# Attention and two MLPs on one core: the first product of each MLP as seven block products per pair of tiles

## The chip, the core and the metric

The kernel runs on one core of one Trainium2 chip. The core has TensorE (PE in the rows, its weight loads apart as PEld), VectorE (DVE), ScalarE (ACT), GpSimd (POOL) and SyncE (SP, which here only starts DMAs). They share the on-chip memory SBUF; TensorE writes its results to PSUM, eight banks of 512 fp32 columns, which DVE and ACT read. The metric is the device time of one launch in microseconds; lower is better.

## What is computed

Attention over 4 x 8 heads of 576 tokens with rotary positions gives x, 2304 tokens by 512. Two MLPs follow, each with 2048 hidden features:

```python
def _moe_ref(x, w_in, w_out, s, b):
    h = x @ w_in                 # 2304x512 @ 512x2048
    r = np.maximum(h, 0.0)
    g = s * (r * r) + b
    return (g @ w_out).astype(np.float32)

def _moe2_ref(x, w_in, w_out):
    h = x @ w_in
    g = h * (1.0 / (1.0 + np.exp(-1.702 * h)))
    return (g @ w_out).astype(np.float32)
```

All is fp32. Every product of the MLPs is made of three TensorE products: an operand is split in a high part (rounded to the type fp32r, which TensorE reads) and a low part (the rest), and high x high, high x low and low x high are summed in PSUM.

## The kernel before

Every engine has its own program, written out by hand, and engines wait for each other on counting semaphores. The attention of 16 pairs of heads comes first. Tables (PE_ORDER, ACT_ORDER, DVE_ORDER, POOL_ORDER, SP_ORDER) set the order of its steps on each engine; "H@-1" means that step H of pair p stands in round p + 1. A hook `after(s)` of the SP and POOL programs puts further work behind round s; that is where the first weights are loaded (L275, L277) and split (`first_w`, L309 and L288).

The MLPs then run in 192 steps, n = 0 to 191. The 2304 tokens are cut in six chunks C of 384, and for every chunk of every MLP there are 16 steps, one for each 128 hidden features. The attention's result and later the first MLP's lie transposed in `xT`, as four tiles of 128 features. A step has on TensorE:

- `H_step` (L956): 4 input tiles x 3 products = 12 matmuls of 384 columns into one of two PSUM banks (`hps`).
- `Y_step` (L984), two steps later (LAG = 2): in the first MLP 4 x 3 = 12 matmuls of 384 columns, in the second 3 x 3 = 9 of 512 columns, summed over the chunk's 16 steps in banks ACC. Chunks take turns on these banks.

Between the two, `gate` on ACT and `gate_low` on DVE apply the function and split the result in `ghi` and `glo`: relu or sigmoid (L918, L920), square or product (L932, L934), high part (L924, L926), low part (L937, L940). `extras` adds what comes seldom: weights are split once for each MLP (`split_w`, L285 on ACT, L288 on DVE) and kept in SBUF for all six chunks; the next chunk's x is split in steps 5, 7, 9 and 11 (`split_x`, L294 and L297), one tile of 384 each, into the other of two buffers; `evacuate` (L997, L1000) copies a chunk's result to `xT`. GpSimd has nothing to do in the MLPs: it splits the first two weights and the low part of the first x during the attention and ends with `finish` (L538, L542, L545), which normalises a pair's result and writes it to `xT`. Step 0 of H stands inside the last round of the attention, between the two PV products (L651) of the last pair.

## Time and profile before

| | us |
|---|---|
| median of 3 runs | 1119.11 |
| lowest, highest | 1119.0, 1119.51 |
| span of the profiled execution | 1117.4 |

Busy time in the profiled execution: TensorE matmuls 1090.4 us (98%), weight loads 1036.1 (93%), DVE 553.5 (50%), ACT 500.8 (45%), POOL 247.4 (22%). The profiled execution's span runs from the first to the last instruction; the device time is 1.7 us longer. Matmuls overlap in the pipeline, so a row's duration of a matmul says little; what counts is the distance between the starts of two of them. The attention takes the first 315 us, the MLPs the rest, and the trace gives for each instruction its start, its length and, where its engine was idle before, what released it.

### The profile page before, as it was taken

To read this page: it belongs to the slowest core of one execution; us is meant where nothing else is said; L and a number is where in the kernel's file an instruction comes from. 1 tells how busy PE (TensorE), PEld (TensorE's weight loads), DVE (VectorE), ACT (ScalarE), POOL (GpSimd) and SP (SyncE) were. 2 spreads that over 40 slices of the span, in tenths; PEclk is the share of its full clock that TensorE was granted. 3 is DMA by queue.
4 is the path that set the end of the run, shared out by engine and by line. 5 is a ranking of instruction groups with operands and counts; after the bars stand their busy time and mean duration, and the time that the engine had idled before them with its cause. 6 is when DMAs were issued, how large, how long until landed. Compare 5 with 4: busy or idle time off the path is not lost.

```text
span 1117.4 us, 16936 instructions
## 1 busy us (share of the span) xinstructions
PE 1090.4 (98%) x6522; PEld 1036.1 (93%) x6522; DVE 553.5 (50%) x885; ACT 500.8 (45%) x1031; POOL 247.4 (22%) x276
## 2 busy tenths in 40 slices
PE   4899999999999999999999999999999999999998
PEld 4899999999999999999999999999999999999997
DVE  6888888898866333333333356532332323333222
ACT  4888788878755332232332345422322222222222
POOL 6878878895720000000000000000000000000000
PEclk9999999999999999999999999999999999999999
DMA  4555454553243100000000014200000000000000
GB/s 109 126 147 145 128 152 130 147 138 91 69 132 125 37 1 1 1 1 1 1 1 1 1 57 133 76 1 1 29 1 29 1 15 15 1 29 1 29 1 29
DMA packets 59187, 59.47 MB, mean 53 GB/s; under 512 B 13780, under 2 KB 46820, under 8 KB 59108
## 3 DMA queue, kind: packets, MB, share of 16 engines
q1 hardware_dynamic: 58272, 57.90, 18.6%
q8 instruction: 52, 0.85, 0.3%
q10 hardware_dynamic: 836, 0.49, 0.1%
q14 instruction: 27, 0.22, 0.1%
HBM read 35.88 MB, written 4.79 MB: 36 GB/s over the span
## 4 chain that ended last, share of the span: by engine, by line
PE 90%; DVE 4%; ACT 3%; DMA 1%; issue 1%; POOL 1%; SPq 0%; ACTq 0%; POOLq 0%; DVEq 0%
PE psum L956 36%; PE psum L984 36%; PE psum L651 7%; PE psum L605 4%; PE psum L579 4%; ACT E L713 2%; DVE negmax L805 1%; PE psum L681 1%; DVE osum L835 1%; DVE Xlo L815 1%; PE psum L615 0%; PE psum L631 0%; DMA sin<-in_k_sin_dram 0%; PE psum L679 0%; DVE QK L858 0%
## 5 line engine op out<-in xcount | busy, mean ns | idle before, releaser
L956 PE MATMUL psum<-xhi,Wlo 128*128 128x384 f32 x768 | 257.8, 336 | 0.0
L956 PE MATMUL psum<-xhi,Whi 128*128 128x384 f32 x768 | 257.6, 335 | 0.0
L956 PE MATMUL psum<-xlo,Whi 128*128 128x384 f32 x768 | 257.2, 335 | 0.0
L956 PEld LDWEIGHTS psum<-xhi,Whi 128*128 128x128 f32 x768 | 144.2, 188 | 4.2
L956 PEld LDWEIGHTS psum<-xlo,Whi 128*128 128x128 f32 x768 | 144.1, 188 | 4.1
L956 PEld LDWEIGHTS psum<-xhi,Wlo 128*128 128x128 f32 x768 | 144.1, 188 | 0.0
L937 DVE SCALAR_TENSOR_TENSOR glo<-act,sb_sb,ghi 128x384 fp32r<-128x384 f32 x96 | 59.4, 619 | 145.4 <-ACT ghi L924 145.4
L924 ACT ACTIVATE ghi<-act,sb_sb 128x384 fp32r<-128x384 f32 x96 | 59.2, 617 | 157.7 <-PE psum L984 150.3
L940 DVE TENSOR_TENSOR glo<-act,ghi 128x384 fp32r<-128x384 f32 x96 | 53.6, 559 | 152.0 <-ACT ghi L926 152.0
L984 PE MATMUL psum<-ghi,Whi 128*128 128x384 f32 x384 | 128.3, 334 | 0.0
L984 PE MATMUL psum<-glo,Whi 128*128 128x384 f32 x384 | 128.3, 334 | 0.0
L984 PE MATMUL psum<-ghi,Wlo 128*128 128x384 f32 x384 | 128.3, 334 | 0.0
L926 ACT CAST ghi<-act 128x384 fp32r<-128x384 f32 x96 | 49.3, 514 | 157.0 <-PE psum L984 157.0
L934 DVE TENSOR_TENSOR act<-psum,act 128x384 f32<-128x384 f32 x96 | 53.5, 558 | 124.1 <-ACT act L920 124.1
L984 PE MATMUL psum<-Wlo,ghi 128*128 128x512 f32 x288 | 113.9, 396 | 0.0
L984 PE MATMUL psum<-Whi,glo 128*128 128x512 f32 x288 | 113.7, 395 | 0.0
L984 PE MATMUL psum<-Whi,ghi 128*128 128x512 f32 x288 | 111.9, 389 | 0.0
L920 ACT ACTIVATE act<-psum 128x384 f32<-128x384 f32 x96 | 47.2, 492 | 129.6 <-PE psum L956 129.6
L713 ACT ACTIVATE E<-psum,negmax 128x576 f32<-128x576 f32 x128 | 94.7, 745 | 13.6 <-DVE negmax L805 13.3
L805 DVE TENSOR_REDUCE negmax<-psum 128x1 f32<-128x576 f32 x128 | 91.2, 752 | 14.7 <-PE psum L579 14.1
L932 DVE SCALAR_TENSOR_TENSOR act<-act,sb_sb 128x384 f32<-128x384 f32 x96 | 60.3, 628 | 76.4 <-ACT act L918 76.4
L579 PE MATMUL psum<-QK,Q 128*128 128x320 f32 (+1 forms) x512 | 86.3, 309 | 9.1 <-ACT E L713 6.9
(107 smaller groups left out, 1844.4 us busy)
## 6 DMA issues: line engine op xcount, KB each, us to landing
Q<-QK SPq DMA_DIRECT2D x60, 144.0 KB, 3.1
QK<-QK SPq DMA_DIRECT2D x30, 288.0 KB, 3.4
wraw<-in_moe_w_in_dram SPq DMA_DIRECT2D x32, 256.0 KB, 2.9
wraw<-in_moe_w_out_dram SPq DMA_DIRECT2D x32, 256.0 KB, 3.1
vraw<-in_v_dram SPq DMA_DIRECT2D x32, 128.0 KB, 2.3
raw<-in_q_dram SPq DMA_DIRECT2D x30, 128.0 KB, 2.9
raw<-in_k_dram SPq DMA_DIRECT2D x30, 128.0 KB, 2.8
inv_row<-inv_dram SPq DMA_DIRECT2D x16, 144.0 KB, 2.9
```

The lines of the kernel that those rows point to most:

```text
L579: mm = pe.matmul(ps[:, a:b], Q[h][p % 2][:, at:at + P], QK[h][p % 2][:, part, c:c + b - a], start=part == 0, stop=part == 1)
L651: mm = pe.matmul(ps[:, a:b], V[h][:, j, :, :].rearrange("p a d -> p (a d)"), x, start=j == 0 and n == 0, stop=j == NM and n == 1, skip_gro ...
L713: act.activation(E[p % 2][:, j, h, :], row(banks("S", p, h, j), h), ACT.Exp, bias=negmax[p % 2][:, c:c + 1], accum_out=sums[p % 2][:, c:c ...
L805: dve.tensor_reduce(negmax[p % 2][:, c:c + 1], row(banks("S", p, h, j), h), AX_X, ALU.max, negate=True).then_inc(max_done, 1)
L924: act.activation(ghi[n % 2][:], a[:], ACT.Identity, bias=sb_sb[:, 1:2]).then_inc(g_hi, 1)
L926: act.copy(ghi[n % 2][:], a[:]).then_inc(g_hi, 1)
L932: dve.scalar_tensor_tensor(a[:], a[:], sb_sb[:, 0:1], a[:], ALU.mult, ALU.mult).then_inc(g_done, 1)
L934: dve.tensor_tensor(a[:], hps(n), a[:], ALU.mult).then_inc(g_done, 1)
L937: dve.scalar_tensor_tensor(glo[n % 2][:], a[:], sb_sb[:, 1:2], ghi[n % 2][:].bitcast(F32), ALU.add, ALU.subtract).then_inc(g_lo, 1)
L940: dve.tensor_tensor(glo[n % 2][:], a[:], ghi[n % 2][:].bitcast(F32), ALU.subtract).then_inc(g_lo, 1)
L956: mm = pe.matmul(hps(n), w[i][:, kt * P:(kt + 1) * P], x[C % 2][:, kt, :], start=kt == 0 and j == 0, stop=kt == KT - 1 and j == 2)
L984: mm = pe.matmul(dst, lhsT, rhs, start=i == 0 and j == 0, stop=i == NF - 1 and j == 2)
```

## The change

The first product of an MLP is no longer made tile by tile. The unit is now a window: 256 hidden features by 768 tokens (CH = 2 x 384), with the 512 input features in two halves. So W (256 x 512) and x (512 x 768) are two-by-two blocks, and the four result blocks of 128 x 384 come from seven block products (Strassen's scheme in Winograd's form) in place of eight. There are three chunks of 768 tokens and 8 windows for each, 24 for an MLP and 48 in all.

- TensorE. `product(n, k)`, k = 0 to 6, is 2 x 3 = 6 matmuls of 384 columns, so 42 for a window, where four H steps were 48. Products 0, 1 and 3 start a PSUM bank, the others add on; two banks take turns. `y_part` is the second product for tile a (first 128 features) or tile b (second 128), each in three parts that stand between the products: parts of b of window n - 2 behind products 0, 1, 2, and parts of a of window n - 1 behind products 3, 4, 5. In the first MLP the transposed result of 4 x 768 columns is laid over six banks of 512, so a tile has 4 x 3 matmuls of 512 and 4 x 3 of 256 columns; in the second MLP 6 x 3 of 512. All six banks belong to the one running chunk.
- Recombining. ACT copies out P1 (product 0), U2 (product 2 on top of 0) and P5 (product 3); DVE adds the blocks to these: `block_11` (product 1 + P1), h_b (product 4's bank + P5) and h_a (product 5's bank + U2). The fourth block is read by ACT and DVE from product 6's bank. The functions then run on 768 columns at a time.
- Weights are no longer kept. For each window SP loads 512 KB of w_in and 512 KB of w_out, again for each chunk. GpSimd makes four sums of weight blocks (`w_sum`, 4 x 256), ACT makes the high parts (`win_high` 768 + 1024, `wout_high` 1024) and GpSimd the low parts (`win_low` 768 + 1024, `wout_low` 1024).
- x. GpSimd makes four sums of x blocks for the next chunk (`x_sum`, 768 each) in windows 1 to 4 of a chunk. ACT and DVE split all seven operands of 768 in the chunk's last window (k = 0 to 5) and in the next one's first (k = 6). There is one buffer for them.
- At the end of the attention POOL does the sums and high parts for window 0 and the first two x operands, SP no longer loads the third and fourth weights, and `product(0, 0)` and `product(0, 1)` take the place of H step 0. The ACT splits `xhi@-8` and the POOL splits `xlo@-9` of rounds 8 to 12 are gone.

The core of the diff, the engines' programs for a window:

```diff
-                      "hi10@-1 hi11@-1 hi12@-1 hi13@-1 xhi@-8 split@-1 evac0@-1 exp00@1 exp01@1 exp02@1 exp03@1 expT@1 "
+                      "hi10@-1 hi11@-1 hi12@-1 hi13@-1 xc02@-1 xc03@-1 wsplit@-1 xc04@-1 evac0@-1 xc05@-1 xc06@-1 exp00@1 exp01@1 exp02@1 exp03@1 expT@1 "
...
+                def first_x(k):
+                    pool.wait_ge(s_done, 2 * NM * (NPAIR - 1))
+                    pool.wait_ge(sT_done, NPAIR - 1)
+                    pool.tensor_tensor(xc_hi[k][:], x_source(0, k), zero[:, :].unsqueeze(2).broadcast_to([P, HK, N]), ALU.add).then_inc(first_x_hi, 1)
+                    pool.wait_ge(first_x_hi, k + 1)
+                    pool.tensor_tensor(xc_lo[k][:], x_source(0, k), xc_hi[k][:].bitcast(F32), ALU.subtract).then_inc(first_x_lo, 1)
...
+                    if s == NPAIR - 4:
+                        pool.wait_ge(x_done, CHUNK_PAIRS)
+                        for step in range(4):
+                            x_sum(pool, 0, step)
+                    if s == NPAIR - 3:
+                        first_w_sums()
+                        first_w_hi()
+                    if s == NPAIR - 2:
+                        win_low(pool, 0)
+                        first_x(0)
+                    if s == NPAIR - 1:
+                        first_x(1)
+                        w_sum(pool, 1)
...
+            def w_sum(pool, m):
+                r = win_raw[m % 2]
+                a11, a12, a22, a21 = [r[:, o:o + BLK] for o in (RAW_A11, RAW_A12, RAW_A22, RAW_A21)]
+                pool.wait_ge(win_in[m % 2], 48 * (m // 2 + 1))
+                need(pool, win_lo_done, m)
+                pool.tensor_tensor(S1, a21, a22, ALU.add).then_inc(w_sum_step, 1)
+                pool.tensor_tensor(S3, a11, a21, ALU.subtract)
+                pool.wait_ge(w_sum_step, 2 * m + 1)
+                pool.tensor_tensor(S2, S1, a11, ALU.subtract).then_inc(w_sum_step, 1)
+                pool.wait_ge(w_sum_step, 2 * m + 2)
+                pool.tensor_tensor(S4, a12, S2, ALU.subtract).then_inc(w_sums, 1)
+            def win_high(act, m):
+                act.wait_ge(w_sums, m + 1)
+                need(act, product_done, 7 * (m - 1))
+                act.copy(win_hi[m % 2][:, 0:3 * BLK], win_raw[m % 2][:, 0:3 * BLK])
+                act.copy(win_hi[m % 2][:, 3 * BLK:7 * BLK], wsum[:]).then_inc(win_hi_done, 1)
+            def win_low(pool, m):
+                pool.wait_ge(win_hi_done, m + 1)
+                pool.tensor_tensor(win_lo[m % 2][:, 0:3 * BLK], win_raw[m % 2][:, 0:3 * BLK], win_hi[m % 2][:, 0:3 * BLK].bitcast(F32), ALU.subtract)
+                pool.tensor_tensor(win_lo[m % 2][:, 3 * BLK:7 * BLK], wsum[:], win_hi[m % 2][:, 3 * BLK:7 * BLK].bitcast(F32), ALU.subtract).then_inc(win_lo_done, 1)
...
+                if k == 0:
+                    need(pe, dve_read, 3 * n)
+                elif k == 1:
+                    need(pe, act_read, 4 * n)
+                    if n > PER_MLP:
+                        pe.wait_ge(last_read, n - PER_MLP)
+                elif k == 2:
+                    pe.wait_ge(act_read, 4 * n + 1)
+                elif k == 3:
+                    pe.wait_ge(dve_read, 3 * n + 1)
...
+                for t in range(HK):
+                    at = (W_OF[k] * HK + t) * P
+                    for i, (w, x) in enumerate(((win_hi, xc_hi), (win_hi, xc_lo), (win_lo, xc_hi))):
+                        mm = pe.matmul(hps(n, k), w[n % 2][:, at:at + P], x[k][:, t, :], start=k in FRESH and t == 0 and i == 0,
+                                       stop=t == HK - 1 and i == 2, skip_group_check=True)
...
+            def keep_first(act, n):
+                need(act, dve_read, 3 * n - 2)
+                act.wait_ge(product_done, 7 * n + 1)
+                act.copy(P1[:], hps(n, 0)).then_inc(act_read, 1)
+            def block_11(dve, n):
+                dve.wait_ge(act_read, 4 * n + 1)
+                dve.wait_ge(product_done, 7 * n + 2)
+                dve.tensor_tensor(h_a[:, 0:N], hps(n, 1), P1[:], ALU.add).then_inc(dve_read, 1)
...
+                    if splits:
+                        for k in (1, 2, 3):
+                            x_split(dve, C + 1, k, False)
+                    dve.wait_ge(act_read, 4 * n + 3)
+                    dve.wait_ge(product_done, 7 * n + 5)
+                    dve.tensor_tensor(h_b[:, N:CH], hps(n, 4), P5[:], ALU.add).then_inc(dve_read, 1)
...
+            def x_split(eng, C, k, hi):
+                if hi:
+                    eng.wait_ge(product_done, 7 * (NJ * C - 1) + k + 1)
+                    if k == 0:
+                        x_ready(eng, C)
+                    if k == 2:
+                        eng.wait_ge(x_summed, C + 1)
+                    eng.copy(xc_hi[k][:], x_source(C, k)).then_inc(x_hi, 1)
+                else:
+                    eng.wait_ge(x_hi, NOPS * C - POOL_OPS + k + 1)
+                    eng.tensor_tensor(xc_lo[k][:], x_source(C, k), xc_hi[k][:].bitcast(F32), ALU.subtract).then_inc(x_lo, 1)
+            def pool_window(pool, n):
+                C, j = n // NJ, n % NJ
+                if n + 1 < WINDOWS:
+                    win_low(pool, n + 1)
+                if C + 1 < 2 * NCH and 1 <= j <= 4:
+                    if j == 1:
+                        pool.wait_ge(x_lo, NOPS * (C + 1) - POOL_OPS)
+                        x_ready(pool, C + 1)
+                    x_sum(pool, C + 1, j - 1)
+                if n + 2 < WINDOWS:
+                    w_sum(pool, n + 2)
+                wout_low(pool, n)
```

What this does to the order of the engines' instructions is shown at three places. In these lists a row is an instruction with its output, inputs and size, and "x2" stands for two alike.

GpSimd from the last V splits of the attention to the first window, before. `sums_eps` is the sum of the last pair's row sums, V and V are high and low parts of the values, `osum` and `xT` are `finish`:

```order
L309 TENSOR_TENSOR Whi<-wraw,zero 128x1024 [waits s_done,prep_t,sT_done,rotated,wraw_in1]
L288 TENSOR_TENSOR Wlo<-wraw,Whi 128x1024 [waits w_hi_done]
L528 TENSOR_TENSOR sums_eps<-sums,eps 128x9 [waits inv_done,expT_done,exp_done]
L518 TENSOR_TENSOR V<-vraw,zero 128x5x64 [waits pv_done,v_in0]
L518 TENSOR_TENSOR V<-vraw,zero 128x5x64 [waits pv_done,v_in1]
L522 TENSOR_TENSOR V<-vraw,V 128x5x64 [waits v_hi] x2
L538 TENSOR_TENSOR osum<-osum,O 128x576 [waits half_done,evac_done]
```

The same stretch of GpSimd after, from the same place:

```order
L1019 TENSOR_TENSOR win_lo0<-win_raw0,win_hi0 128x768 [waits win_hi_done]
L1020 TENSOR_TENSOR win_lo0<-wsum,win_hi0 128x1024
L555 TENSOR_TENSOR xc_hi0<-xT,zero 128x768 [waits sT_done,s_done]
L557 TENSOR_TENSOR xc_lo0<-xT,xc_hi0 128x768 [waits first_x_hi]
L549 TENSOR_TENSOR sums_eps<-sums1,eps 128x9 [waits inv_done,expT_done,exp_done]
L539 TENSOR_TENSOR V0<-vraw,zero 128x5x64 [waits pv_done,v_in0]
L539 TENSOR_TENSOR V1<-vraw,zero 128x5x64 [waits pv_done,v_in1]
L543 TENSOR_TENSOR V0<-vraw,V0 128x5x64 [waits v_hi]
L543 TENSOR_TENSOR V1<-vraw,V1 128x5x64 [waits v_hi]
```

Four instructions now stand ahead of `sums_eps`, where two did. Behind `finish` of the pair before the last, where before only `finish` of the last pair followed, GpSimd has now:

```order
L555 TENSOR_TENSOR xc_hi1<-xT,zero 128x768 [waits sT_done,s_done]
L557 TENSOR_TENSOR xc_lo1<-xT,xc_hi1 128x768 [waits first_x_hi]
L1004 TENSOR_TENSOR wsum<-win_raw1 128x256 [waits win_lo_done,win_in1]
L1005 TENSOR_TENSOR wsum<-win_raw1 128x256
L1007 TENSOR_TENSOR wsum<-wsum,win_raw1 128x256 [waits w_sum_step]
L1009 TENSOR_TENSOR wsum<-win_raw1,wsum 128x256 [waits w_sum_step]
L573 TENSOR_TENSOR osum1<-osum1,O1 128x576 [waits half_done,evac_done]
```

The last round of the attention on ACT, before (O is a PV product's evacuation, Xhi the last transposed scores):

```order
L727 CAST Xhi<-psum 128x512 [waits x_t] x3
L285 CAST Whi<-wraw 128x1024 [waits wraw_in0]
L744 COPY O<-psum 64x576 [waits sum_done,pv_done]
L918 ACTIVATE act<-psum 128x384 [waits h_done,sb_in]
L924 ACTIVATE ghi<-act,sb_sb 128x384 [waits g_done]
L744 COPY O<-psum 64x576 [waits pv_done]
```

and after:

```order
L775 CAST Xhi<-psum 128x512 [waits x_t] x3
L808 CAST xc_hi<-x_sums 128x768 [waits x_t,xQ_t,sT_done,xT_t,s_done,x_summed] x2
L1014 CAST win_hi<-win_raw 128x768 [waits xT_t,w_sums,xQ_t,x_t]
L1015 CAST win_hi<-wsum 128x1024
L808 CAST xc_hi<-x_sums 128x768 [waits x_t,xQ_t,sT_done,xT_t,s_done,x_summed]
L792 COPY O<-psum 64x576 [waits sum_done,pv_done]
L808 CAST xc_hi<-xT 128x768 [waits x_t,xQ_t,sT_done,xT_t,s_done,x_summed]
L808 CAST xc_hi<-x_sums 128x768 [waits x_t,xQ_t,sT_done,xT_t,s_done,x_summed]
L1112 COPY P<-psum 128x384 [waits product_done]
L792 COPY O<-psum 64x576 [waits pv_done]
```

Both evacuations and the first P1 copy (L1112) now stand behind the high part of window 1's weights (L1014), which waits for GpSimd's sums.

DVE in a chunk's last window. Before, the steps that split x had one such instruction among the gates:

```order
L932 SCALAR_TENSOR_TENSOR act<-act,sb_sb 128x384 [waits first_done]
L937 SCALAR_TENSOR_TENSOR glo<-act,sb_sb,ghi 128x384 [waits g_hi]
L288 TENSOR_TENSOR Wlo<-wraw,Whi 128x1024 [waits w_hi_done]
L297 TENSOR_TENSOR xlo<-xT,xhi 128x384 [waits x_hi]
L932 SCALAR_TENSOR_TENSOR act<-act,sb_sb 128x384 [waits first_done]
```

After, the end of that window and the beginning of the next:

```order
L1157 TENSOR_TENSOR xc_lo<-xT,xc_hi 128x768 [waits x_hi]
L1117 TENSOR_TENSOR h_a<-psum,P 128x384 [waits product_done,act_read]
L1278 SCALAR_TENSOR_TENSOR gb_lo<-a_b,sb_sb,gb_hi 128x768 [waits g_hi_b]
L1157 TENSOR_TENSOR xc_lo<-xT,xc_hi 128x768 [waits x_hi]
L1157 TENSOR_TENSOR xc_lo<-x_sums,xc_hi 128x768 [waits x_hi] x2
L1267 TENSOR_TENSOR h_b<-psum,P 128x384 [waits product_done,act_read]
L1157 TENSOR_TENSOR xc_lo<-x_sums,xc_hi 128x768 [waits x_hi]
L1271 TENSOR_TENSOR h_a<-psum,U 128x384 [waits product_done]
L1157 TENSOR_TENSOR xc_lo<-xT,xc_hi 128x768 [waits x_hi]
L1237 SCALAR_TENSOR_TENSOR a_a<-a_a,sb_sb 128x768 [waits act_a]
L1243 SCALAR_TENSOR_TENSOR a_b<-a_b,sb_sb 128x768 [waits act_read]
L1278 SCALAR_TENSOR_TENSOR ga_lo<-a_a,sb_sb,ga_hi 128x768 [waits g_hi_a]
```

Six low parts of x (L1157) now share a window with the gates; three of them stand ahead of the h_b addition (L1267), and one ahead of h_a (L1271).

## Rows read from the trace of the kernel before

**Rows 1.** The page: span, busy time of each engine, granted TensorE clock in 40 slices.
```profile
span 1117.4 us, 16936 instructions
PE 1090.4 (98%) x6522; PEld 1036.1 (93%) x6522; DVE 553.5 (50%) x885; ACT 500.8 (45%) x1031; POOL 247.4 (22%) x276
PEclk9999999999999999999999999999999999999999
```
**Rows 2.** Timeline of TensorE, first MLP: start us, length us, instruction; 24 matmuls apart.
```profile
364.99 0.33 PE L984 MATMUL psum<-ghi,Whi 128*128 128x384 f32 x1
...
369.15 0.33 PE L984 MATMUL psum<-ghi,Whi 128*128 128x384 f32 x1
```
**Rows 3.** Chain of work in order, second MLP: start us, length us; one step apart.
```profile
720.83 2.10 PE psum L956 x12
725.02 2.10 PE psum L956 x12
```
**Rows 4.** Timeline of TensorE, last PV but one: matmuls of 256 columns.
```profile
302.51 0.28 PE L651 MATMUL psum<-XThi,V 128*128 128x256 f32 x1
302.63 0.28 PE L651 MATMUL psum<-XTlo,V 128*128 128x256 f32 x1
```
**Rows 5.** Groups by line and shape: count, busy us, mean ns, then idle before.
```profile
L924 ACT ACTIVATE ghi<-act,sb_sb 128x384 fp32r<-128x384 f32 x96 | 59.2, 617 | 157.7 <-PE psum L984 150.3 <-DVE act L932 7.4
L815 DVE TENSOR_TENSOR Xlo<-psum,Xhi 128x512 fp32r<-128x512 f32 x128 | 82.8, 683 | 4.8 <-ACT Xhi L727 4.7
L285 ACT CAST Whi<-wraw 128x1024 fp32r<-128x1024 f32 x30 | 31.1, 1038 | 0.2 <-DMA wraw<-in_moe_w_out_dram 0.2
L294 ACT CAST xhi<-xT 128x384 fp32r<-128x384 f32 x48 | 24.2, 504 | 0.0
L937 DVE SCALAR_TENSOR_TENSOR glo<-act,sb_sb,ghi 128x384 fp32r<-128x384 f32 x96 | 59.4, 619 | 145.4 <-ACT ghi L924 145.4
L934 DVE TENSOR_TENSOR act<-psum,act 128x384 f32<-128x384 f32 x96 | 53.5, 558 | 124.1 <-ACT act L920 124.1
L288 DVE TENSOR_TENSOR Wlo<-wraw,Whi 128x1024 fp32r<-128x1024 f32 x30 | 36.9, 1229 | 10.3 <-ACT Whi L285 10.3
L297 DVE TENSOR_TENSOR xlo<-xT,xhi 128x384 fp32r<-128x384 f32 x44 | 24.3, 553 | 0.0
L288 POOL TENSOR_TENSOR Wlo<-wraw,Whi 128x1024 fp32r<-128x1024 f32 x2 | 4.8, 2397 | 0.2
L297 POOL TENSOR_TENSOR xlo<-xT,xhi 128x384 fp32r<-128x384 f32 x4 | 4.1, 1026 | 0.0
```
**Rows 6.** Timelines of GpSimd and DVE where both work on SBUF, and each alone.
```profile
317.59 2.17 POOL L542 TENSOR_TENSOR xT<-osum,inv_row 128x512 f32<-128x512 f32 x1
318.51 1.65 DVE L932 SCALAR_TENSOR_TENSOR act<-act,sb_sb 128x384 f32<-128x384 f32 x1
...
308.75 1.30 POOL L542 TENSOR_TENSOR xT<-osum,inv_row 128x512 f32<-128x512 f32 x1
322.93 0.61 DVE L932 SCALAR_TENSOR_TENSOR act<-act,sb_sb 128x384 f32<-128x384 f32 x1
```
**Rows 7.** Timelines of GpSimd, DVE and TensorE at the end of the attention.
```profile
298.19 1.90 POOL L309 TENSOR_TENSOR Whi<-wraw,zero 128x1024 fp32r<-128x1024 f32 x1
304.12 0.22 DVE L828 RECIPROCAL inv<-sums_eps 128x9 f32<-128x9 f32 x1
305.57 1.70 POOL L522 TENSOR_TENSOR V<-vraw,V 128x320 fp32r<-128x320 f32 x2
307.24 1.43 POOL L538 TENSOR_TENSOR osum<-osum,O 128x576 f32<-128x576 f32 x1
310.12 0.34 PE L956 MATMUL psum<-xhi,Whi 128*128 128x384 f32 x1
314.98 0.42 PE L956 MATMUL psum<-xhi,Whi 128*128 128x384 f32 x1
```
**Rows 8.** Stages by window: busy us of each engine, granted clock, DMA share, GB/s.
```profile
25.00:30.00 5.00, 4.40 (x22) 3.85 (x22) 3.29 (x5) 3.24 (x9) 4.78 (x6) 0.66 0.55 138
```

More of the change, by code:

```diff
@@ L687, in first_H @@
                     if p == NPAIR - 1:
-                        H_step(pe, 0)
+                        product(pe, 0, 0)
+                        product(pe, 0, 1)
                 def IT_job(p, _, __):
@@ new lines, in fused_kernel, with store @@
+            last_out = x_sums[:, :, :, :].rearrange("p a b n -> p (a b n)").rearrange("p (u d) -> p u d", u=UT)
+            def store(eng, C, bank):
+                at = C % NCH * CH
+                done, value = ev_of(C, bank)
+                eng.wait_ge(done, value)
+                rows = out[at + bank * P:at + (bank + 1) * P, :]
+                if C == 2 * NCH - 1:
+                    eng.dma_start(rows, last_out[:, bank, :]).then_inc(stored, 16)
+                    return
+                for b, col, m, tok, size in YT_PIECES:
+                    if b == bank:
+                        eng.dma_start(rows[:, col:col + size], xT[:, m, at + tok:at + tok + size]).then_inc(stored, 16)
@@ L1062, in _ @@
                     attention_gpsimd(pool)
+                    for n in range(WINDOWS):
+                        pool_window(pool, n)
                 @block.tensor
```

647 lines of the change are left out of this document (380 added, 267 removed).

## The prediction

> **What bounds the kernel now.** Start at the page: TensorE is busy 98% of 1117.4 us at the full granted clock (9 in every slice: 2.4 GHz); GpSimd, at 22%, works only in the attention [rows 1]. Busy time counts overlapping matmuls, so next look at starts. In the first MLP 24 matmuls of 384 columns take 369.15 - 364.99 = 4.16 us, 0.1733 us each, with no gap [rows 2]. A step of the second MLP takes 4.19 us [rows 3]: 12 x 0.1733 = 2.08, so its 9 matmuls of 512 take 2.11, or 0.234 each. ACT and DVE are not late: their gates L924, L934 and L937 sat idle 157.7, 124.1 and 145.4 us, each waiting for its predecessor and in the end for TensorE [rows 5]. TensorE's own matmuls set the time from 310.12 us on, and there is not even a gap where the attention hands over to the MLPs [rows 7]. What is saved on TensorE is saved on the clock, as long as nothing else becomes late.
>
> **What TensorE saves.** The first products fall from 48 to 42 matmuls per window: 48 windows x 6 x 0.1733 = **49.9 us**. In the first MLP the second product changes shape: 48 matmuls of 384 (8.32 us per window) become 24 of 256 and 24 of 512. A 256 takes 0.12 [rows 4]. From 256 and 384, 128 more columns cost 53 ns, which puts a 512 at 0.227; the steady 512s took 0.234 [rows 3]. So 8.32 to 8.50 us: a loss of 0 to 4.3 us in 24 windows. I take 4.2, since the steady row is the nearer one. The second MLP's second product is the same. Net **-45.7** (bounds -49.9 and -45.7). A window is then 7.28 + 8.4 = 15.7 us.
> The Trainium skill, "TensorE: Matmul & The Clock Gate", section "Back-to-back issue gap", has N / 2.4 ns plus 2.5 ns for a gap. These rows show 13 ns more than N / 2.4. By the page the net would be 288 x 0.1625 = -46.8.
>
> **What the other engines get in a window.** From [rows 5], one more element per partition costs 0.83 ns on ACT (1038 - 504 over 640), 1.06 on DVE, 2.14 on GpSimd (2397 - 1026 over 640). So 768 elements take ACT 0.82 (0.94 with bias; a relu as a copy), DVE 0.96 (1.02 with a scalar), GpSimd 1.85.
> ACT: three copies and one relu of 384, relu 384 and 768, two high parts of g, 1.86 + 1.04 for weights: about 8 us, and 4.9 more in a chunk's last window. Fits in 15.7.
> DVE: three additions from PSUM at 0.56 and four gates at 1.02: 5.8 us, 5.8 more in the last window.
> GpSimd: four sums at 0.75, low parts 1.85 + 2.40 + 2.40: 9.7 us; 11.5 in the four windows with an x sum. Fits alone.
> DMA: 1 MB per window is 67 GB/s; [rows 8] show 138, so it is hidden, two windows ahead.
>
> **DVE and GpSimd together.** While GpSimd's L542 ran, DVE's L932, whose inputs both lie in SBUF, took 1.65 us, not 0.61, and L542 2.17, not 1.30 [rows 6]. The lengths fit turns: one instruction of one engine at a time. DVE work with a PSUM operand shows nothing of it: L815, 128 times beside a GpSimd that was busy in most of the attention, took 0.683 for 512, just what L934's 0.558 for 384 leads to [rows 5]. The Trainium skill says so too ("GPSIMD Engine Reference", "Key points": GpSimd shares its SBUF interfaces with VectorE, which matters for DVE instructions with two SBUF inputs); the trace agrees.
> So per window 9.7 + 4.1 = 13.8 us share one resource, 15.6 with an x sum, against 15.7. Close, but is it on the path? I laid out one window, t = 0 at product 0. P1 must be out by 5.2 (product 2), block_11 by 7.3 (product 3), h_a of the window before by 0. Product 6 ends at 15.7. GpSimd starts win_low at 4.0, when ACT has done relu 0.65, high part a 1.6, P1 2.0 and win_high 3.9, and ends wout_low at 15; an x sum makes that 16.5 to 17. The gate of tile a is ready at 15.1 and then waits for wout_low to 16.5: 1.8 us later all told. P1 then comes at 3.2 instead of 2.0. Still ahead of 5.2, and next window the phases have swapped. **Plain windows: 0** in the first MLP. In the second, DVE must read product 6's bank (last_read) behind that gate, at 2.3 to 2.7, and product 1 is due at 2.4: 8 such windows x 0.1 to 0.3 = **+1** (bounds 0 and 5).
> A chunk's last window has 9.7 + 9.9 = 19.6 us of shared work in 15.7. Taking turns, DVE's six x parts interleave with GpSimd's: h_b is out at 14.3 (due 14.6), h_a at 15.8 (due 15.7), and wout_low pushes the next gate to 4.3 us after the next window's start. ACT waits there for sq_a, so P1 is out at 5.6 (due 5.2) and block_11 at 8 (due 7.3): 1 us at each of the first three handovers. At the two inside the second MLP last_read comes at 4.9 instead of 2.4: 2.5 us each. **+8** for five handovers (bounds 0, if the turns cost nothing, and 25, if each x part waits for a full 2.40).
>
> **The end of the attention.** This costs most, and has nothing to do with steady load.
> 1. From 298.19 GpSimd has 1.90 + 2.40 = 4.3 us of weights to split, then `sums_eps`; DVE's inv runs at 304.12 [rows 7]. Now win_low(0) 4.25 and first_x(0) (1.5 + 1.85) stand there: 7.6 us, `sums_eps` at 305.8, inv at 306.1. The low parts behind it slip, and PV0 with them: +1.7.
> 2. GpSimd goes on without rest: the V parts (two lows in 1.70 [rows 7], two highs, at most 0.85 each like the lows; I take 0.7) to 309.1, finish to 312.2 (1.43 [rows 7], 1.30 [rows 6] and a small rest), first_x(1) to 315.7, w_sum(1) to 319 or, with turns, 319.6. Product 1 needs first_x(1): it waits from 312.9 to 316, and PV1 behind it ends at 320 (before: 314.98).
> 3. ACT stands at win_high(1), which waits for w_sum(1): 319.6, done 321.5. Behind it, in order: three x parts, both evacuations, P1 at 325. TensorE's product 2 waits for P1: idle from 320 to 325.
> 4. Products 2 to 6 end at 330.6 (P5 also waits for w_out, loaded only after PV1). GpSimd: evac1 at 325.6, finish to 329.6, win_low(1) to 333.9: window 1 waits 3.3 us. It waits again, 1.3, for wout_low(0), and ends at 346.9.
> Without waits the same work would end at 310.12 + 2.08 + 2.75 + 5.2 + 11.5 = 331.7. The difference is **+15** us (bounds 8, if w_sum(1) is not late and only steps 1 and 4 remain, and 20). TensorE idles 3 to 5 us three times. In [rows 8] the granted clock fell to 0.66, part of a stretch at 1.2 GHz, at the attention's start; a repeat would add up to 2 us, within these bounds. The removed xhi and xlo of rounds 8 to 12 stood beside TensorE work: 0.
> The end of the kernel: six tiles are stored, not three, but the last copy and store are as before: 0 (up to +2).
>
> **Sum** against the profiled span: 1117.4 - 45.7 + 1 + 8 + 15 = 1095.7; with the 1.7 us that lie around the span, **1097.5 us** against 1119.1, some 2% less.
>
> **Rivals.**
> A. The turns hardly cost anything, because DVE's instructions slip between GpSimd's. For: the turns rest on one overlap, and GpSimd is idle for some 4 us of a window in which gates can pass. Against: in that one overlap both lost about 1 us [rows 6]. Price: handovers and x sums 0 to 2, attention's end 12: 1117.4 - 45.7 + 13 + 1.7 = 1086.
> B. Slower than before. GpSimd, not TensorE, paces the windows with an x sum and the last ones. Mechanism: ACT's win_high waits for the sums and GpSimd's win_low for win_high, so a round of GpSimd can't start before 4.0; with 12.6 us behind it, it ends at 16.6. If an instruction in the shared interface costs 25% more than its turn (2.9 us), a round passes the 18 to 19 us at which product 0's wait for win_low and P1 slip, and 25 of 48 windows grow by 2 us or more, the other 23 by little: +50 on the forecast, 1147. It decides from about 0.5 us per window, averaged over all 48: that takes back the 22 us gain. For: 15.6 of 15.7 leaves nothing. Against: 1.8 us of slack at P1.
> C. The same turns, but an x part or gate on average waits out a win_low of 2.40, not a sum of 0.75: handovers of 4 us and 2 for the x-sum windows: 1117.4 - 45.7 + 15 + 20 + 2 + 1.7 = 1110.
> D. The change saves less than it says: a wait before each product opens a gap of 0.05 us, 336 x 0.05 = 17: 1114. Against: before, each step's waits opened none [rows 2].
>
> **How the numbers follow.** Forecast (1091 to 1105) 50%; A (1080 to 1091) 20%; C 12%; D 4%; B 14%. Of D 1 and of B 2 lie within 0.2% of before. 0.2% (2.2 us) is what a measurement of this kernel can tell from no change. Faster 85%, same 3%, slower 12%. The range 1082 to 1114 leaves out most of B and the lowest of A.
>
> **What would show it.** Right: starts of product matmuls 0.173 apart and windows of 15.6 to 15.8 us in the middle of chunks; TensorE idle of about 5 us before product 2 of window 0, released by ACT's P1, with ACT idle at win_high for GpSimd's w_sum; idle before product 0 of window 1 for win_low; small idles at windows 8, 16, 24, 32 and 40, larger in the last two, released by last_read; L542-like stretching of DVE's 768 gates beside GpSimd. Wrong: product 0 of many windows waiting for win_low, x parts of GpSimd above 1.85 us throughout, or 512s of the first MLP away from 0.227 to 0.234.

## The result, and the profile after

The changed kernel takes **1091.93 us** (median; 1091.24 to 1092.2), the kernel before 1119.05 beside it: a ratio of 0.9761, with a 95% interval of 0.9747 to 0.9775. The forecast was 1097.5 us in a range of 1082 to 1114. The profiled execution took 1091.24 us, with a span of 1089.0 against a forecast 1095.7.

The page of the changed kernel, the parts that answer to [rows 1]:

```profile
span 1089.0 us, 17061 instructions
PE 1046.7 (96%) x6234; PEld 963.4 (88%) x6234; DVE 686.8 (63%) x827; ACT 635.2 (58%) x1124; POOL 799.1 (73%) x634
...
PE   4899999999968999999999999999999999999998
...
POOL 6878787878779976688677876777866776676640
PEclk9999999999999999999999999999999999999999
```

TensorE is still the busy engine. GpSimd went from 22% to 73% of the span. The twelfth slice (299 to 327 us), the end of the attention, has the 6: there TensorE stands.

The chain of waits of the changed kernel in the first MLP (start, length, what; product 6 of one window and product 0 of the next make one piece of 12 matmuls):

```profile
362.67 2.10 PE psum L1068 x12
...
378.38 2.10 PE psum L1068 x12
...
692.51 2.10 PE psum L1068 x12
...
724.72 2.08 PE psum L1068 x12
```

From one window to the next it is 15.71 us, and from 362.67 to 692.51, 21 windows, 329.84 / 21 = 15.707: no window of the first MLP, neither one with an x sum nor one at a handover, waits for anything. From 692.51 to 724.72 are two windows: 32.21, 0.8 more than 2 x 15.71. So windows take what the forecast's 7.28 + 8.4 = 15.7 says, and the waits that remain lie at the start of the second MLP, inside it and at the end of the attention.

The same view at the second chunk pair of the second MLP, where a handover costs:

```profile
820.21 3.08 DVE a_a L1235
823.29 0.48 DVE a_b L1240
823.77 0.14 issue
823.90 1.30 PE psum L1068 x6
```

The gate of tile a takes 3.08 us here, then comes last_read (a_b L1240), and TensorE's product 1 has waited for that. The turns (VectorE and GpSimd, both on SBUF, one instruction at a time) are seen in VectorE's and GpSimd's timelines (start, length, instruction). The first row is the same gate one window earlier, with GpSimd idle:

```profile
803.76 0.96 DVE L1235 TENSOR_TENSOR a_a<-h_a,a_a 128x768 f32<-128x768 f32 x1 [0.91 <-ACT a_a L1161]
...
820.18 3.11 DVE L1235 TENSOR_TENSOR a_a<-h_a,a_a 128x768 f32<-128x768 f32 x1
```

0.96 alone, 3.11 beside GpSimd. GpSimd's win_lo (L1020) and wout_lo (L1024), 2.40 each when alone [rows 5], stretch too, the first to 3.09 on average, the second to 2.52. The page's groups of GpSimd (count, busy us, mean ns, idle before):

```profile
L1019 POOL TENSOR_TENSOR win_lo<-win_raw,win_hi 128x768 fp32r<-128x768 f32 x48 | 91.2, 1899 | 181.7 <-ACT win_hi L1015 181.7
...
L1020 POOL TENSOR_TENSOR win_lo<-wsum,win_hi 128x1024 fp32r<-128x1024 f32 x48 | 148.5, 3094 | 0.0
L1024 POOL TENSOR_TENSOR wout_lo<-wout_raw,wout_hi 128x1024 fp32r<-128x1024 f32 x48 | 121.1, 2523 | 13.4 <-ACT wout_hi L1225 13.4
```

The end of the attention, TensorE's timeline, the rows with idle time before them (in brackets: us of it, and what ended it):

```profile
315.33 0.69 PE L1068 MATMUL psum<-xc_hi,win_hi 128*128 128x384 f32 x1 [4.05 <-POOL xc_lo L557]
...
323.30 0.41 PE L1068 MATMUL psum<-xc_hi,win_hi 128*128 128x384 f32 x1 [2.53 <-ACT P L1112]
...
333.04 0.44 PE L1068 MATMUL psum<-xc_hi,win_hi 128*128 128x384 f32 x1 [1.99 <-POOL win_lo L1020]
...
340.40 0.50 PE L1096 MATMUL psum<-ga_hi,wout_hi 128*128 128x512 f32 x1 [1.95 <-POOL wout_lo L1024]
```

and ScalarE's at the same place:

```profile
318.26 0.84 ACT L1014 CAST win_hi<-win_raw 128x768 fp32r<-128x768 f32 x1 [8.92 <-POOL wsum L1009]
...
322.68 0.47 ACT L1112 COPY P<-psum 128x384 f32<-128x384 f32 x1
```

These are the forecast's steps 2, 3 and 4 ([rows 7] show the same place before), in their order and with their releasers: product 1 for first_x(1), ScalarE 8.92 us at win_high(1) for the sums and P1 behind it, window 1 for win_low(1), and the wait for wout_low(0). Window 1 ends at 348.0, forecast 346.9.

### The profile page after: what moved, and what is told of

Read it like the earlier page. It is cut to its first block, busy times and chain, and to the rows that moved or that the text cites. A ratio compares the mean times of both kernels' runs of the same rounds, so it can differ in the third digit from the quotient of the medians.

```text
span 1089.0 us, 17061 instructions
## 1 busy us (share of the span) xinstructions
PE 1046.7 (96%) x6234; PEld 963.4 (88%) x6234; DVE 686.8 (63%) x827; ACT 635.2 (58%) x1124; POOL 799.1 (73%) x634
## 4 chain that ended last, share of the span: by engine, by line
PE 81%; DVE 8%; ACT 4%; POOL 4%; issue 2%; DMA 1%; ACTq 0%; SPq 0%; POOLq 0%; DVEq 0%
PE psum L1096 35%; PE psum L1068 30%; PE psum L698 6%; PE psum L626 4%; PE psum L652 4%; ACT E L761 2%; DVE negmax L860 1%; DVE xc_lo L1157 1%; DVE Xlo L870 1%; DVE osum L890 1%; DVE a_a L1235 1%; PE psum L728 1%; DVE QK L913 1%; POOL win_lo L1020 0%; DMA sin<-in_k_sin_dram 0%
## 5 line engine op out<-in xcount | busy, mean ns | idle before, releaser
L1068 PE MATMUL psum<-xc_hi,win_hi 128*128 128x384 f32 x672 | 227.6, 339 | 12.5 <-POOL xc_lo L557 4.0
L1068 PE MATMUL psum<-xc_lo,win_hi 128*128 128x384 f32 x672 | 227.0, 338 | 0.0
L1068 PE MATMUL psum<-xc_hi,win_lo 128*128 128x384 f32 x672 | 226.3, 337 | 0.0
L1019 POOL TENSOR_TENSOR win_lo<-win_raw,win_hi 128x768 fp32r<-128x768 f32 x48 | 91.2, 1899 | 181.7 <-ACT win_hi L1015 181.7
L1020 POOL TENSOR_TENSOR win_lo<-wsum,win_hi 128x1024 fp32r<-128x1024 f32 x48 | 148.5, 3094 | 0.0
L1068 PEld LDWEIGHTS psum<-xc_hi,win_hi 128*128 128x128 f32 x672 | 126.9, 189 | 23.9 <-issue 8.1
L1068 PEld LDWEIGHTS psum<-xc_lo,win_hi 128*128 128x128 f32 x672 | 126.9, 189 | 8.0
L1024 POOL TENSOR_TENSOR wout_lo<-wout_raw,wout_hi 128x1024 fp32r<-128x1024 f32 x48 | 121.1, 2523 | 13.4 <-ACT wout_hi L1225 13.4
L1068 PEld LDWEIGHTS psum<-xc_hi,win_lo 128*128 128x128 f32 x672 | 127.0, 189 | 0.0
L1267 DVE TENSOR_TENSOR h_b<-psum,P 128x384 f32<-128x384 f32 x48 | 26.7, 556 | 148.1 <-PE psum L1068 148.1
L870 DVE TENSOR_TENSOR Xlo<-psum,Xhi 128x512 fp32r<-128x512 f32 x128 | 82.6, 680 | 4.6 <-ACT Xhi L775 4.5
L1271 DVE TENSOR_TENSOR h_a<-psum,U 128x384 f32<-128x384 f32 x48 | 26.7, 556 | 83.5 <-PE psum L1068 83.5
```

The source lines that it names most:

```text
L870: dve.tensor_tensor(Xlo[:, h, j, 0:MAIN], banks("X", p, h, j), Xhi[:, h, j, 0:MAIN].bitcast(F32), ALU.subtract).then_inc(et_lo, 1)
L1019: pool.tensor_tensor(win_lo[m % 2][:, 0:3 * BLK], win_raw[m % 2][:, 0:3 * BLK], win_hi[m % 2][:, 0:3 * BLK].bitcast(F32), ALU.subtract)
L1020: pool.tensor_tensor(win_lo[m % 2][:, 3 * BLK:7 * BLK], wsum[:], win_hi[m % 2][:, 3 * BLK:7 * BLK].bitcast(F32), ALU.subtract).then_inc(wi ...
L1024: pool.tensor_tensor(wout_lo[m % 2][:], wout_raw[m % 2][:], wout_hi[m % 2][:].bitcast(F32), ALU.subtract).then_inc(wout_lo_done, 1)
L1068: mm = pe.matmul(hps(n, k), w[n % 2][:, at:at + P], x[k][:, t, :], start=k in FRESH and t == 0 and i == 0, stop=t == HK - 1 and i == 2, sk ...
```

## The experiments

Of the changed kernel each was one variation; times are medians beside the 1091.9 us of the changed kernel. The kernel before, run again beside each group of these runs, had medians of 1119.05, 1118.38, 1118.49 and 1118.13, and the intervals of the ratios are about 1.5 us to either side. So a difference of two medians of 1 to 1.5 us shows nothing by itself. The traces are finer, because they let the kernel be cut in stages. Two stages, from the starts of matmuls in TensorE's timelines (us):

| version | product 0 of window 0 to product 6 of window 1 | from there to product 6 of window 46 |
|---|---|---|
| changed kernel | 36.73 (310.07 to 346.80) | 709.83 |
| product 0 twice | 36.73 | 752.85 |
| GpSimd's last work twice | 39.10 | 734.71 |
| most low parts left out | 36.69 | 705.39 |
| read ahead of the gate, last windows | 36.70 | 708.84 |
| read ahead of the gate, all windows | 36.70 | 708.11 |
| first order | 35.34 | 709.63 |
| second order | 32.64 | 709.63 |
| both orders | 31.40 | 709.68 |
| both, two moves, early read | 31.06 | 708.11 |
| the same, down weights first | 31.11 | 708.11 |

What was not touched comes out the same within 0.2 us, so differences of a stage can be read to that. Ahead of these stages the executions differ by themselves: product 0 of window 0 starts at 310.07 in the changed kernel and at 310.93, 310.37, 310.62 and 311.90 in four versions with the same attention.

The expectations for the first two count 32 windows, and 24 matmuls in a product; this was a slip of mine. There are 48 windows, and a product has 6 matmuls (two blocks of the contraction, three terms). What they would have said with the right counts stands under each.

**One product twice.** Product 0's matmuls run a second time; the first pass is overwritten.

```
-                for t in range(HK):
+                for t in [t for _ in range(2 if k == 0 else 1) for t in range(HK)]:
```

> The 24 matmuls of product 0 are run twice in each of the 32 windows (the first pass is overwritten), all else as in the changed kernel; the output is the same. Theory (TensorE's own work sets every window's 15.7 us, and a matmul of 384 columns costs 0.1733 us): 32 windows x 24 x 0.1733 = +133 us against the changed kernel (1091.9), so 1225. Rival (GpSimd's 12.1 us of busy time and its waits, or the gates on VectorE, hold part of the window's 15.7 us): a window of MLP1 has TensorE idle that the added 4.16 us first fills, so less than 133, some 100 to 125, a time of 1192 to 1217.

Measured: 1136.05 us, +44.1. With the right count the theory says 48 x 6 x 0.1733 = +49.9. The number that was on record (+133) has no value. The chain of waits:

```profile
381.32 3.14 PE psum L1068 x18
...
398.07 3.14 PE psum L1068 x18
```

A window of the first MLP is now 16.75 us long, 1.04 more than 15.71, which is all of the six matmuls. In the second MLP it is 16.68. So nothing but TensorE sets these windows. The 5.8 us that are missing from 49.9 are waits that the longer windows swallow: from product 6 of window 1 to that of window 46 it grew by 43.0 instead of 46.8 (the turns' waits in the second MLP), and windows 0 and 1 took their 12 further matmuls, 2.1 us, without growing at all: 36.73 us with them and without. So TensorE does not set the time of these two windows. This run also gives the balance: with eight products' work per window, as before the change, the kernel takes 17.7 us more than before. That is what the change costs apart from the product that it saves, net of those 5.8 us.

**GpSimd's last work twice.** The low part of the down weights is formed twice in every window, the second behind the first.

```
-                pool.tensor_tensor(wout_lo[m % 2][:], ..., ALU.subtract).then_inc(wout_lo_done, 1)
+                pool.tensor_tensor(wout_lo[m % 2][:], ..., ALU.subtract).then_inc(lo_once, 1)
+                pool.wait_ge(lo_once, m + 1)
+                pool.tensor_tensor(wout_lo[m % 2][:], ..., ALU.subtract).then_inc(wout_lo_done, 1)
```

> GpSimd forms the low part of the second product's weights (512 columns) twice in each window, the second behind a wait for the first: 1.3 us more alone, about 3.1 when it takes turns with a copy of VectorE. Theory (the turns cost the windows nothing because GpSimd stands idle about 4 us in each of 15.7, and only the moves from one pair of chunks to the next feel a slower gate): 0 to +4 us against the changed kernel, 1092 to 1096. Rival (GpSimd and VectorE together stand close behind TensorE, so that each turn more is paid): at least 1.3 us in each of 32 windows, +42 us, 1134; with all taken in turns +99.

Measured: 1118.69 us, **+26.8**: neither. The theory's +4 falls. The added work is 2.4 us alone and 3.1 in turns (the expectation's 1.3 was wrong too: this instruction has 1024 elements), so if all were paid it would be +115 to +149. The chain of waits in a window with an x sum:

```profile
359.34 2.53 POOL win_lo L1020
361.87 2.37 POOL win_lo L1021
...
364.29 1.71 issue
...
370.98 2.38 POOL wout_lo L1025
...
373.43 2.39 POOL wout_lo L1027
375.82 2.52 POOL win_lo L1020
```

Here GpSimd alone makes the window, without a pause: 375.82 - 359.34 = 16.48 us (the 1.71 of "issue" are its x sum, and the weight sums stand behind it). Without the added 2.46 this is 14.0, against TensorE's 15.7. So in a window with an x sum GpSimd stands only **1.7 us** behind TensorE in the changed kernel, not the 4 us that its idle time suggested: that idle time (181.7 us, all of it for ScalarE's win_hi) is partly used up when GpSimd comes late, since it then no longer waits. But these windows are not where most of the time goes. Of the 27.4 us by which the span grew, windows 2 to 5, the first with x sums, have 3.1, and six windows at the handovers (7 and 8, 15 and 16, 23 and 24: the last of a chunk and the first of the next) have 13.3. Windows 7 and 8 grew by 2.65 and 2.26 us, together twice the added 2.46: there all of it is paid. (The rest: the start 2.4, other windows of the first MLP 4.1, the second MLP 4.5.) The chain of waits through window 7 and into window 8:

```profile
431.53 3.24 DVE a_a L1240
434.77 2.14 DVE a_b L1246
...
438.78 2.50 DVE xc_lo L1160
...
441.75 2.59 DVE gb_lo L1281
...
453.08 3.09 DVE a_a L1240
```

Window n is here what ends with product 6 of window n. Most of the chain is VectorE's gates and x parts, stretched beside GpSimd; from 459.99 it is GpSimd's win_low again. So at the handovers of the first MLP, where the changed kernel lost nothing, the two engines together had next to no reserve left. A plain window without an x sum in the middle of a chunk pays nothing (15.71 for window 6, 15.64 in the second MLP from 1005.67 to 1021.31). Rival B of the prediction, which named the windows with an x sum and the last ones, is a real mechanism with its threshold 1.7 us away in the first and close to nothing in the second; the change stays below it.

**Most of GpSimd's low parts left out.** From window 2 on each of the two low parts of the first product's weights is cut to 2 columns. Left out is the rest of these low parts, so the output is not the reference's.

```
-                pool.tensor_tensor(win_lo[m % 2][:, 0:3 * BLK], ...)
-                pool.tensor_tensor(win_lo[m % 2][:, 3 * BLK:7 * BLK], wsum[:], ...)
+                w1, w2 = (3 * BLK, 4 * BLK) if m < 2 else (2, 2)
+                pool.tensor_tensor(win_lo[m % 2][:, 0:w1], ...)
+                pool.tensor_tensor(win_lo[m % 2][:, 3 * BLK:3 * BLK + w2], wsum[:, 0:w2], ...)
```

> From window 2 on GpSimd forms only 2 columns of each of the two low parts of the first product's weights (left out: the rest of those low parts, so the products use stale low weights), which takes about 4.4 us of GpSimd work (up to 5.1 in turns) out of each window; TensorE's matmuls are the same. Theory (what is left of the change's cost of turns is the two 1.15 us waits for last_read inside MLP2, 0.55 at its start, and some 0.15 us in each of its first windows): -3 to -4 us against the changed kernel, 1088 to 1089. Rival 1 (turns slow nothing that TensorE waits for): 0. Rival 2 (the turns also stretch TensorE's own instructions): the window of MLP1 falls below 15.70 us, -10 us or more.

Measured: 1087.03 us, **-4.9**, a little more than the theory's 3 to 4. The same gate at the same handover:

```profile
802.48 0.96 DVE L1236 TENSOR_TENSOR a_a<-h_a,a_a 128x768 f32<-128x768 f32 x1 [0.91 <-ACT a_a L1162]
...
818.91 0.96 DVE L1236 TENSOR_TENSOR a_a<-h_a,a_a 128x768 f32<-128x768 f32 x1
```

It takes 0.96 both times, and the second MLP runs from 724.17 to 1052.61 in 21 windows of exactly 15.64. Its windows of the first MLP stay at 15.71: the turns don't touch TensorE's own instructions, which refutes rival 2. By groups VectorE's gates of tile a (L1237 and L1235) fall from a mean of 1993 and 1810 ns to 1054 and 958. Against this the changed kernel lost 3.6 us from 724.72 to 1056.79 and 0.8 in the two windows before. So what comes back with these low parts is 4.4 us (the stage of 709.83 is 705.39), although VectorE's busy time falls by 61.6 us (686.8 to 625.2): the turns with these low parts stretched its work fourteen times as much as they cost.

**The read ahead of the gate.** First at the last window of a pair of chunks of the second MLP, then in every window of it: VectorE reads product 6's block before it multiplies tile a.

```
+                    if second(m) and m % NJ == NJ - 1:
+                        dve.wait_ge(act_read, 4 * n)
+                        dve.tensor_tensor(a_b[:, 0:N], hps(m, 6), a_b[:, 0:N], ALU.mult).then_inc(last_read, 1)
                     dve.wait_ge(act_a, n)
```

> At the last window of each pair of chunks of MLP2, VectorE reads product 6's block for the gate of tile b (the read that product 1 of the next window waits for) ahead of the gate of tile a instead of behind it; everything else is as changed. Theory (the 1.15 us waits of TensorE come from the gate of tile a, 2 to 3 us in turns with GpSimd, that stands ahead of this read): both waits and the 0.55 at window 25 go, -2.5 to -2.8 us, 1089.2. Rival (the read waits as long for the sigmoid on ScalarE, or the later gate of tile a then holds the down product): 0, or up to +2 us.

Measured: 1090.74 us, -1.2; the stage of the windows fell by 1.0. The expectation's 0.55 at window 25 could not go, since the edit reaches only windows behind the second MLP's own chunk ends. The waits had gone from windows 32 and 40, but turned up at the next:

```profile
839.25 0.41 PE L1068 MATMUL psum<-xc_hi,win_hi 128*128 128x384 f32 x1 [0.42 <-DVE a_b L1244]
```

> As e4_last_read, but in every window of MLP2: VectorE reads product 6's block (last_read) ahead of the gate of tile a. In the trace of e4 the wait of 0.5 us had only moved on by a window, and products of 1.20 to 1.24 us instead of 1.04 stood in the windows after each handover. Theory (each of these is the gate of tile a, in turns with GpSimd, ahead of last_read): all windows of MLP2 take 15.64 us and both handovers and the start of MLP2 cost nothing, so -3.5 to -4 us against the changed kernel (1091.9), 1088.2, the same MLP2 as where GpSimd's low parts are left out. Rival (the later gate of tile a now holds ScalarE's high part and with it the down product): -1 to +3 us.

Measured: 1090.36 us, -1.6 (the stage of the windows: -1.7): less than half of the theory's. All plain windows of the second MLP take 15.64 and its start costs nothing, but the handovers still cost 1.34 each (788.27 to 836.53, three windows, 48.26 instead of 46.92). The chain of waits through the first of them:

```profile
816.36 2.91 DVE xc_lo L1157 x2
...
822.43 0.56 DVE a_b L1235
822.99 2.20 DVE a_a L1238
...
825.95 0.48 ACT P L1112
826.43 0.14 issue
826.57 1.28 PE psum L1068 x6
```

Product 1 is on time now. But the gate of tile a, behind the early read, still takes 2.20 us beside GpSimd, ScalarE waits for it before its copy P1, and product 2 for P1: the expectation's rival, at the handovers alone. Ahead of it stand VectorE's x parts, one of 3.16 us beside win_low and the two of the row at 816.36, 1.45 each beside the sums, which have made everything late by then. So "the gate ahead of last_read" was the place where the delay showed, and only in part its cause: taking the low parts away removed it, reordering moved it.

**The end of the attention.** Orders of the same work. The first puts ScalarE's evacuation and first steps of window 0 ahead of the weights' split, and one of VectorE's additions earlier:

```
-  xc02@-1 xc03@-1 wsplit@-1 xc04@-1 evac0@-1 xc05@-1
+  xc02@-1 xc03@-1 evac0@-1 first@-1 wsplit@-1 xc04@-1 xc05@-1
```

> Only the order of ScalarE and VectorE in the last steps of attention differs: ScalarE evacuates chunk 0 and splits the first window's operands ahead of the high weights of window 0 (the high part it keeps last), and VectorE does its first operand ahead of the low part of operand 4. GpSimd is untouched. Theory (the end of attention costs 16 us because GpSimd's single file of operand 1, the sums of window 1 and the low weights stands last at TensorE's 4.05, 1.99 and 1.95 us waits): little, 0 to -3 us against the changed kernel, 1089 to 1092. Rival (ScalarE and VectorE set the end of attention): -5 us or more.

Measured: 1090.16 us, -1.8, as the theory has it (five runs from 1089.52 to 1092.07; by the traces the start is 1.4 shorter). The second takes operand 1 off GpSimd (POOL_OPS from 2 to 1) and puts the sums of window 1 ahead of the last outputs:

```
-    POOL_OPS = 2
+    POOL_OPS = 1
...
-    POOL_ORDER = order("rot1@3 eps@0 V0@0 V1@0 vlo0@0 vlo1@0 finish@-1 rot0@4")
+    POOL_ORDER = order("rot1@3 eps@0 V0@0 V1@0 vlo0@0 vlo1@0 ws@0 finish@-1 rot0@4")
```

> The operand of product 1 of the first window is split by ScalarE and VectorE instead of GpSimd, and GpSimd forms the weight sums of window 1 right behind its low parts of V, ahead of the last outputs of attention. Theory (GpSimd's file of work is what the first products wait for): the 4.05 us wait for xc_lo goes, and of the 2.5 us wait for P1 and the two waits for low weights (3.9 us) some 2 to 4 go: -5 to -8 us against the changed kernel, 1084 to 1087. Rival (the same work, 1.0 us each on ScalarE and VectorE, stands just as late there): 0 to +3 us.

Measured: 1085.62 us, **-6.3**. The waits of 4.05 and 2.53 us are gone; in their place stand 1.16 and 1.75, for P1 and block_11. By the traces the start is 4.1 us shorter and the windows 0.2; the medians have 2 us more, of which 1.6 is that the changed kernel was profiled in its quickest execution and this one in its slowest. So what these two moves take off GpSimd's single file is between a quarter and two fifths of the 16 us. They were made together, and which of them brought it isn't shown.

> The orders of e5 and e6 together, without the other moves of e8. If their gains add (1.8 and 6.3 us): 1083.8, as e8, and then the two further moves of e8 and the early last_read, 1.5 us alone, brought nothing together. If they do not add (both shorten the same wait for P1 and the same file of GpSimd): 1085 to 1086.

Measured: 1084.82 us, -7.1. The two orders alone have 8.1, but the 1.0 between is within what medians differ by. By the traces they add: the start is 1.4 shorter with the first, 4.1 with the second and 5.3 with both.

> The orders of e5, e6 and e9 together, and two moves more: in window 0 ScalarE copies P5 ahead of the high part of the down weights, and GpSimd forms the low weights of window 1 ahead of the last outputs of attention. If the causes add: -3.7 (MLP2), -6.5 (operand 1 and weight sums off GpSimd's file), -2 (order), -2 (low weights of window 1): -10 to -14 us against the changed kernel, 1078 to 1082. If the waits at the end of attention stand behind one another, so that each removal uncovers the next: -6 to -9, 1083 to 1086.

Measured: **1083.83 us**, -8.1, a ratio of 0.9689 to the kernel before (0.9676 to 0.9703): the fastest version of this study. It falls short of the 1078 to 1082 that the expectation has if the causes add, but two of its terms were never measured to be so large: the second MLP's 3.7 was 1.6 to 1.7 (read ahead of the gate, above), and the two further moves brought little: product 6 of window 1 starts at 341.3, against 341.5 without them and 347.0 in the changed kernel. The gain against the version before, 1.0 by the medians and 1.6 by the spans, is the early last_read in the second MLP. What stands there now, in TensorE's timeline:

```profile
323.37 0.66 PE L1074 MATMUL psum<-xc_hi,win_hi 128*128 128x384 f32 x1 [3.17 <-DVE h_b L1278]
...
333.23 0.65 PE L1102 MATMUL psum<-ga_hi,wout_hi 128*128 128x512 f32 x1 [2.58 <-POOL wout_lo L1030]
```

> As e8_full, but in window 0 GpSimd forms the low part of the down weights ahead of the weight sums of window 2. In e8 TensorE waits 2.6 us for these low weights at 330.6, and after the wait its first matmuls of 512 columns run 0.43 us apart instead of 0.23 (granted clock 0.82 to 0.84 there). Theory (this wait is GpSimd's order alone): -2.5 to -3.5 us against e8 (1083.8), 1080.3 to 1081.3, more than the wait itself since the clock then stays up. Rival (the sums of window 2, 2.4 us later, hold the high weights of window 2 and ScalarE behind them): -1 to +1 us.

Measured: 1085.14 us, +1.3 against the version before; both stages are as long as there (31.11 and 708.11), so no gain, and the 1.3 is not shown to be a loss. The wait for wout_lo went, and one as long came:

```profile
336.50 0.44 PE L1074 MATMUL psum<-xc_hi,win_hi 128*128 128x384 f32 x1 [2.60 <-ACT U L1207]
```

The rival holds: GpSimd's sums of window 2, now behind wout_low, keep ScalarE at win_high(2), and its copy U2 behind that. Whether another order of these 30 us would do better was not tried.

## Why the prediction was right, point by point

**What TensorE saves: right.** Starts 0.1733 apart, windows of 15.71 and 15.64, and 1.04 us for a product (product twice). The size of a 512 was 1% off: (15.71 - 7.28 - 24 x 0.12) / 24 = 0.231 in the first MLP and (15.64 - 7.28) / 36 = 0.232 in the second, not 0.234. The changed kernel's loss by the new shapes is then 24 x 24 x (0.231 + 0.12 - 2 x 0.1733) = 2.5, not 4.2, and the second MLP gained about 1.6 us that the sum didn't have (its 36 matmuls of 512 per window took 0.234 before). Together this was some 3.3 us of the difference.

**Plain windows and x-sum windows: right in the first MLP, 0.** In the second, five windows of 15.80 to 15.83 at its start, so about 0.8 us for a forecast of 1.

**The handovers: too dear.** This is the term of the sum that was mis-sized. Forecast 3 x 1 + 2 x 2.5 = 8; measured 0 at the two handovers within the first MLP, 0.8 at the start of the second, and 1.4 at each of the two inside it, 3.6 in all. The hand-made schedule had the right engines, order and releaser (gate of tile a, then last_read, then product 1), but reckoned everything about 1 us too late: h_a was due at 15.7 and forecast at 15.8, and came at 14.9. The x parts took 3.2 us only where they met a win_low, and 0.95 to 1.5 elsewhere. With the first windows of the second MLP the turns cost 4.4 us for a forecast of 9.

**The end of the attention: right in mechanism; that the size fits so well is partly luck.** +15 forecast, 16 measured. Steps were off in both directions. Step 1 was wrong, and cost nothing: GpSimd reached the low parts 1.5 us earlier than reckoned, and PV0 started at 307.33, as before (307.38). Step 2 had TensorE idle from 312.9 to 316; it stood 4.05 us up to 315.33. Step 3 was 2.5 us instead of 5, since the sums came at 318.2, not at 319.6, and product 2 started at 323.30, 1.7 us before the forecast's 325. From there to the end of window 1 it took 24.7 us, not 21.9: small waits for h_a (0.45 and 0.61) and matmuls at half rate stood there, the latter named in the working as up to 2 us within the bounds and put at nothing in the sum. They took 3 us of TensorE's time, but as far as the traces tell none of the kernel's (below).

**The sum.** Forecast 1095.7, span 1089.0: the difference of -6.7 is made up of the turns (-4.6), the 512s (-3.3) and the end of the attention (+1.1), to 0.1 us. Against the device time the miss is 5.6: the time around the span was 2.2 us in the profiled execution, not 1.7, and that execution was the quickest of four (1095.7 + 1.7 is also 1097.4, not 1097.5).

**The rivals.** A (turns cost nothing, 1086) is refuted by the 4.9 us that came back with the low parts, but was nearer than it looked: the truth lies halfway between the forecast and A. B (GpSimd paces, 1147) did not come, but the doubled low part shows its mechanism 1.7 us away in windows with an x sum, and at the first MLP's handovers nearer still. C and D (1110 and 1114) are refuted by the windows of 15.71 and 15.64, C also by handovers of 0 to 1.4 us where it had 4.

## What to carry to other kernels

When an idle engine is given work, its idle time in the new profile is not its reserve: it may idle because it waits for its predecessor in a loop in which it is one link. Double one of its instructions and see which windows grow, stage by stage; here 4 us of idle time were 1.7 us of reserve in windows with an x sum, and hardly any at the first MLP's handovers, which had shown no wait at all. And when work is moved onto one engine's single file, price the place where that file starts (here the last 40 us of the attention, 16 us lost) apart from the steady windows, which lost little: of the 8 us that the study gained beyond the change, the traces put 5.7 there and 1.7 in the second MLP, and 4.1 of the 5.7 came from taking one operand off that file and moving window 1's sums ahead in it.
